# A fused attention and two MLPs on one core: q transposes one tick later, and the last down products moved into the next MLP

## The reference, cut to what matters

```python
# q, k, v: (4 batches, 8 heads, 576 tokens, 64); all fp32
out_up    = repeat(softmax_attention(mean4(q), mean4(k), mean4(v)), 4)   # pooled by 4 tokens
out_local = softmax_attention(q, k, v, mask=|i - j| < 4)                 # band of 7 keys
x = (out_up + out_local).reshape(2304 tokens, 512)
h = x @ w_in                      # 512 -> 2048
g = s * relu(h) ** 2 + b
x = g @ w_out                     # 2048 -> 512
out = ((x @ w_a) * (x @ w_b)) @ w2   # 512 -> 1536 -> 512
```

## Time and profile before

| | us |
|---|---|
| median of 3 runs | 975.58 |
| the profiled execution, its own time | 975.64 |
| its span, first to last instruction | 973.8 |
| PE matmuls busy | 951.3 |
| PE weight loads busy | 898.5 |
| DVE busy | 611.1 |
| ACT busy | 474.5 |
| POOL busy | 202.0 |

### The profile page before, as it was taken

The page is one execution under the profiler, slowest core; times in us unless marked ns, Lnnn a source line. Parts: engine busy times, 40 slices in busy tenths (PEclk is TensorE's granted clock), DMA queues, the critical chain, the costliest instruction groups (busy, mean ns, idle before and its releaser), DMA issues.

```text
span 973.8 us, 18322 instructions
## 1 busy us (share of the span) xinstructions
PE 951.3 (98%) x6902; PEld 898.5 (92%) x6902; DVE 611.1 (63%) x1087; ACT 474.5 (49%) x1112; POOL 202.0 (21%) x216
## 2 busy tenths in 40 slices
PE   6899999999999999999999999999999999999997
PEld 5799999999999999999999999999999999999996
DVE  5788655655555556555547666666856667766642
ACT  4677554545554445454434544444634345644432
POOL 2200211001210011200012033333333333333310
PEclk8599999999999999999999999999999999999999
DMA  8346220111300122101041142222442222422201
GB/s 199 104 136 164 65 59 20 45 45 43 88 21 20 48 64 67 44 19 44 14 154 34 50 137 66 66 66 66 135 143 79 67 66 66 130 66 65 75 24 66
DMA packets 129352, 71.41 MB, mean 73 GB/s; under 512 B 63248, under 2 KB 120304, under 8 KB 129264
## 3 DMA queue, kind: packets, MB, share of 16 engines
q1 hardware_dynamic: 128224, 69.94, 25.0%
q10 hardware_dynamic: 1040, 0.29, 0.1%
HBM read 60.76 MB, written 9.44 MB: 72 GB/s over the span
## 4 chain that ended last, share of the span: by engine, by line
PE 88%; ACT 6%; DVE 3%; issue 2%; DMA 1%; SPq 1%; POOL 0%; ACTq 0%; DVEq 0%
PE bank L736 27%; PE bank L686 19%; PE bank L672 18%; PE bank L752 15%; ACT sml L795 3%; PE bank L572 2%; PE bank L636 2%; PE bank L619 1%; PE bank L629 1%; PE bank L548 1%; DMA natk<-in_k 1%; ACT smp L786 1%; PE bank L603 1%; PE bank L566 1%; ACT kT L774 1%
## 5 line engine op out<-in xcount | busy, mean ns | idle before, releaser
L736 PE MATMUL bank<-wx 128*128 128x384 f32 x1512 | 287.4, 336 | 0.6 <-ACT u L977 0.6
L736 PEld LDWEIGHTS bank<-wx 128*128 128x128 f32 x1512 | 267.1, 188 | 14.6 <-ACT u L977 0.9
L686 PE MATMUL bank<-g_hi,wx 128*128 128x288 f32 x1024 | 232.1, 302 | 0.0
L672 PE MATMUL bank<-wx 128*128 128x288 f32 x1536 | 226.9, 296 | 0.5 <-ACT relu L889 0.5
L672 PEld LDWEIGHTS bank<-wx 128*128 128x128 f32 x1536 | 211.7, 189 | 0.7 <-ACT relu L889 0.7
L1236 POOL TENSOR_TENSOR raw<-raw 128x256 f32<-128x256 f32 x144 | 143.3, 1013 | 302.9 <-DVE wx L1156 263.4
L686 PEld LDWEIGHTS bank<-g_hi,wx 128*128 128x128 f32 x1024 | 171.4, 188 | 5.3 <-issue 5.2
L752 PE MATMUL bank<-wx 128*128 128x512 f32 x648 | 173.4, 394 | 0.8 <-DVE wx L1156 0.8
L686 PE MATMUL bank<-g_lo,wx 128*128 128x288 f32 x512 | 151.5, 296 | 0.0
L752 PEld LDWEIGHTS bank<-wx 128*128 128x128 f32 x648 | 119.3, 188 | 17.2 <-DVE wx L1156 1.5
L1112 DVE SCALAR_TENSOR_TENSOR g_lo<-relu,b_col,g_hi 128x288 fp32r<-128x288 f32 x128 | 70.6, 552 | 80.4 <-ACT g_hi L894 80.4
(11 more groups left out here) (70 smaller groups left out, 858.8 us busy)
## 6 DMA issues: line engine op xcount, KB each, us to landing
raw<-in_moe_w_b SPq DMA_DIRECT2D x72, 128.0 KB, 2.3
raw<-in_moe_w_a SPq DMA_DIRECT2D x72, 128.0 KB, 2.3
raw<-in_moe_w_out SPq DMA_DIRECT2D x36, 256.0 KB, 2.8
vnat<-in_v SPq DMA_DIRECT2D x32, 144.0 KB
o_transposed<-o_sb SPq DMA_DIRECT2D x8, 576.0 KB, 3.4
o_raw<-o_transposed SPq DMA_DIRECT2D x6, 768.0 KB, 6.3
out<-y SPq DMA_DIRECT2D x18, 256.0 KB, 2.3
natq<-in_q SPq DMA_DIRECT2D x63, 72.0 KB, 2.1
```

What stands on the lines that cost most here:

```text
L672: mm = nc.tensor.matmul(HB[:, 0:HALF], wi(w, kd, f), xs(x, c % 2)[:, kd], start=(kd == 0 and j == 0), stop=(kd == KD - 1 and j == 2))
L686: mm = nc.tensor.matmul(ACC[o][:, 0:HALF], wo(w, f, o), g[:, slot % GB, :], start=(f == 0 and j == 0), stop=(f == F1 - 1 and j == 2))
L736: mm = nc.tensor.matmul(dst, left(w, n, a, kd), right(x, i)[:, kd * HC:(kd + 1) * HC], start=(opens and kd == 0 and m == 0), stop=(kd == K ...
```

## The change

Three things are changed. The ticks of `turn_q` and `take_q` (-4) and of `sum_q` (-3) become one later for the units from 4 on; the ticks of the units 0 to 3 stay. The last `down_matmuls` of the first MLP (slot 127) are issued after product 4 of the second MLP's step 0, and both `take_acc` of the last chunk follow the `u3` copy and the `c22` sum of that step. The overlay is laid out anew: the split products lie at columns 0 to 3071 of `wx`, and the buffers of `last` begin at 3072 (`split_room` keeps the place below them).

```diff
+LAST_DOWN = 4
...
+        sb(last, "split_room", [P, 8 * HC])
         p1_sb, u2_sb, u3_sb, c11_sb, c22_sb, c12_sb = [sb(last, name, [P, HC])[:] for name in
...
-        p_hi, p_lo = split_at(8 * HC + 3 * DM), split_at(12 * HC + 3 * DM)
+        p_hi, p_lo = split_at(0), split_at(4 * HC)
...
     # PE, attention(g)
-                for u in at_tick(g, 1, -4, TURN_SKEW):
+                for u in at_tick(g, 1, -3, TURN_SKEW):
                     turn_q(u)
...
     # PE, end of the first MLP
             down_matmuls(NCH - 1, F1 - 2)
-            down_matmuls(NCH - 1, F1 - 1)
...
             for n in range(STEPS):
                 for i in range(N7):
                     product(n, i)
+                    if n == 0 and i == LAST_DOWN:
+
+                        down_matmuls(NCH - 1, F1 - 1)
...
     # ACT, attention(g)
-                for u in at_tick(g, 1, -4, TURN_SKEW):
+                for u in at_tick(g, 1, -3, TURN_SKEW):
                     take_q(u)
...
-            take_acc(NCH - 1)
...
                 nc.scalar.activation(u3_sb, X_BANK, ACT.Copy).then_inc(u3_taken, 1)
+                if n == 0:
+                    take_acc(NCH - 1)
...
     # DVE, attention(g)
-                for u in at_tick(g, 2, -3, TURN_SKEW):
+                for u in at_tick(g, 2, -2, TURN_SKEW):
                     sum_q(u)
...
-            take_acc(NCH - 1)
...
                 nc.vector.tensor_tensor(c22_sb, Y_BANK, u3_sb, ALU.add).then_inc(c22_ready, 1)
+                if n == 0:
+                    take_acc(NCH - 1)
```

## The result

| | before | after |
|---|---|---|
| median of 4 runs, us | 975.38 | 986.27 |
| lowest to highest | 974.59 to 975.6 | 983.44 to 986.67 |
| profiled execution, its own time | 975.64 | 983.44 |

The changed kernel is slower by a ratio of 1.0107 (95% interval 1.0087 to 1.0127). The forecast was 983.2 us, with a range of 979.5 to 988. The profiled execution lies on the forecast, at 983.44; the other three lie 2.8 to 3.2 us above it.

A forecast was written before the change was run, and what follows sets the result against it. PE's matmuls, busy 951.3 of 973.8 us, were taken to bound the kernel. The terms 5.6 - 4.5 + 6.0 + 1.2 - 0.7 = +7.6 us on 975.64 gave 983.2 us, range 979.5 to 988.

The forecast's parts named there:

- No keys, 12 x 0.47: In 12 periods without keys, `turn_local` waits 0.47 us for ACT's q copy, now queued behind `g_hi`: +5.6 us.
- With keys, 11 x -0.41: In 11 periods with keys, `turn_q` no longer waits for ACT's copy of k, at 0.01 us lost: -4.5 us.
- Chunk 0, +6.0: Units 6 to 8: q copies behind `g_hi` and weight splits stall `turn_local` 2.39, 2.39 and 1.25 us, together +6.0 us.
- Units 4 and 5, +1.2: End of boot stage: unit 4's later q copy and sum delay scores, `g_hi` and the next up matmuls: +1.2 us.
- The seam, -0.7: Second MLP, step 0: the 12 moved down matmuls cover product 5's wait for ACT's `u3` copy: -0.73 us.
- The overlay, zero: New layout of the buffers: only addresses change, no instruction and no new wait is added: zero.
- The lag: From the end of ACT's copy to the first transpose that waited for it: 0.14 us, at 16 stalls.
- The other figure, 0.05: Lag seen at the seam; if matmuls begin before weight loads complete, it holds at 16 stalls: 1.4 us less, 981.8.
- the clock falls in a stall: Rival: at the 2.39 us stalls of units 6 and 7 PE drops to 1.2 GHz: 985.7 or 988.2 us; chance 0.12.
- The rival on the other side, no stall at `turn_local`: Rival: ACT's q copy is done in time, leaving only the gains and the boot's 0.7 us: 971.1 us; chance 0.04.
- The seam's rival: Late step 3 weights hold product 5 of step 1, losing the 0.7 us and more: 983.9 to 984.9; chance 0.08.
- The argument that transposes and dense matmuls on both sides keep the clock up: At the stalls of units 6 and 7: the point held against the clock's fall, which had chance 0.12.

The follow-up runs named there:

- The profile with two falls: The changed kernel measured again with no edit: median 986.46 us (ratio 1.0102); its profiled execution took 985.42 us.

## Why the prediction was right, and where it was short

**No keys, 12 x 0.47.** Right in place and count. PE's timeline of a later period, from the up matmuls at which the chain to `g_hi` begins to `turn_local`, first after and then before:

```profile
...
176.76 1.75 PE L674 MATMUL bank<-wx 128*128 128x288 f32 x12
...
185.46 0.68 PE L621 MATMUL bank<-ident,sml 96*102 96x96 f32 x6 [0.28 <-ACT qT L783]
...
```

```profile
...
186.82 1.75 PE L672 MATMUL bank<-wx 128*128 128x288 f32 x12
...
195.07 0.66 PE L619 MATMUL bank<-ident,sml 96*102 96x96 f32 x6
...
```

That is 185.46 - 176.76 = 8.70 us after and 195.07 - 186.82 = 8.25 us before: 0.45 us. Alone the term measures 4.7 us (0.40 us each), not 5.6.

**With keys, 11 x -0.41.** Right in place and count; 4.0 us measured, 4.5 forecast.

**Chunk 0, +6.0.** The stalls were sized well. From unit 4's `turn_local` to unit 8's the first profile needs 119.97 - 50.40 = 69.57 us, and the kernel whose three copies stay early 114.08 - 49.97 = 64.11: 5.5 us for the three stalls. The profile with two falls needs 122.70 - 50.06 = 72.64, which is 8.5 us more. The medians give 8.8 us. So the forecast has the stalls, and lacks what the clock adds behind them.

**Units 4 and 5, +1.2.** Right, by the trace. From the values of unit 3 to the up matmuls of slot 2, which before start at 50.37, first before and then after:

```profile
...
38.35 0.75 PE L629 MATMUL bank<-ptp,vd 72*64 72x72 f32 x8 [0.55 <-ACT ptp L801]
...
```

```profile
...
38.01 0.75 PE L631 MATMUL bank<-ptp,vd 72*64 72x72 f32 x8 [0.55 <-ACT ptp L805]
...
51.13 1.83 PE L674 MATMUL bank<-wx 128*128 128x288 f32 x12
...
```

That is 50.37 - 38.35 = 12.02 us and 51.13 - 38.01 = 13.12 us: 1.1 us. With the early copy and the late sum it was 12.71, so 0.7 of it comes from the sum and 0.4 from the copy.

**The seam, -0.7.** The wait went as forecast (0.75 us). The median gained 0.4 us, which is inside the noise. The late store takes 0.24 us back, which I had priced at nothing and bounded at 1 us.

**The overlay, zero.** Not tested by itself; inside the seam's -0.4 us nothing of it shows.

**The lag.** The 0.14 us held. The other figure, 0.05, doesn't follow from the rule that was weighed: it puts the difference down to the weight load, and most of the lag passes before the load begins.

**The failed term.** Summed up as measured, the parts are 4.7 - 4.0 + 5.5 + 1.1 - 0.4 = 6.9 us, where the forecast has 7.6; its errors lie on both sides and partly cancel. Two falls add 3.1 us, which makes 10.0, against 10.3 and 10.9 us measured for the changed kernel. The forecast of 983.2 us is thus one for an execution in which the clock doesn't fall, and that the profiled one took 983.44 is in part luck. The median, 986.27, lies above the 985 that the sum with its own spread allowed, and in the range only because that reached up to 988 for the clock. The step that failed is the rival "the clock falls in a stall", which had a chance of 0.12 and a price of at least 2.5 us for one fall. Both later profiles with the long stalls show it, behind both of them, at 1.5 us each, and seven of the changed kernel's eight executions took 985.4 us or more. The prediction's own sign of being wrong, a clock under 1.00 after 50 us, is there in them. I took 5 us at the lower level from the boot stage; here the clock is back after 3.4 us. Its place (the stalls that the copies of units 6 and 7 cause) was right; its chance was much too low, and each fall was priced too high.

The rival on the other side, no stall at `turn_local`, was wrong for this kernel and right for the one whose copy stays early: 971.1 us by its working, 971.51 measured. The seam's rival did not come: product 5 of step 1 was not held by more than tenths.

The argument that transposes and dense matmuls on both sides keep the clock up was wrong. The falls came behind idle stretches of 2.2 us with ten small transposes after them, once behind one of 1.7 us, and none is seen where the stretch was removed or filled. Whether the transposes matter wasn't tested. Whether the clock falls differs between executions: not at all in the first profile, twice in the second, three times in that of the ticks alone. Why one execution keeps it and another doesn't is open.

## What to carry to other kernels

When a step is moved by a slot, ask on each engine separately what it is now queued behind. Here PE's transpose gained 4 us by coming later, and the same move on ACT put the copy behind an instruction that waits for DVE, and behind two weight splits. With ACT's copy left in its old place the kernel is 0.4% faster than before, and not 1.1% slower. And when a change opens a stall of 2 us in dense matmul work, it is worth asking whether the clock falls behind it: here that added 1.5 us to a stall of 2.4 us, in some executions and not in others. A single profile, which may be one without a fall, doesn't tell; the times of the other executions gave the hint.

## What was not expected of the hardware

The clock fell behind an idle stretch of only 2.2 us followed by ten small transposes, though PE had been busy for 13.9 of the 14 us before (50 to 64 us of the second profile), and stayed at half for about 3.4 us: 1.5 us lost each time. With thirty-six added matmuls of 144 columns in two such stretches the profiled execution kept the pace of one without a fall, and the median was 2.3 us lower. And in that profile the granted clock reads 1.00 even where the transposes ran at half pace, so the reading should be set beside the length of a known instruction before it is used.
